# Moving a weight unit ahead of two others and a square ahead of a normalisation in a fused attention and mixing kernel

## The chip, the cores and the metric

The kernel runs on one core of a Trainium2 chip. Its engines are TensorE (matrix products, PE in the profile), VectorE (DVE), ScalarE (ACT), GpSimd (POOL) and SyncE (SP, which here only issues loads and stores). Each runs its own list of instructions in order, and they wait for each other through semaphores. The metric is the time of one execution on the device in microseconds; the median of three is given.

## The reference

Three parts follow one another. All of it is in float32.

```
scores = q @ k.T / sqrt(64); masked to a window of 32 keys (4 heads)
         or to every 4th of 128 keys (4 heads); attn = softmax; x = attn @ v
x_prev = x shifted by one token
xk = mu_k * x + (1 - mu_k) * x_prev ;  xr = mu_r * x + (1 - mu_r) * x_prev
k = relu(xk @ w_k) ; v = (k * k) @ w_v ; x = sigmoid(xr @ w_r) * v
u = x + (x.T @ U @ V).T ;  out = u + relu(u @ w_ch1) @ w_ch2
```

There are 4 batches of 576 tokens, 8 heads of 64, a width of 512, a hidden width of 1024 in the second part and 2048 in the third.

## The kernel before

A float32 product is made of three products of a format that TensorE takes faster: each operand is split into a high part and a low part (the rest), and high times high, high times low and low times high are added up. `three` (L1200) issues them. ScalarE makes most high parts, VectorE or GpSimd the low ones.

The attention is cut into 8 parts `k` of 256 or 320 tokens, and each part into 4 pairs of heads `p`. A pair goes through four steps: A transposes q and k (VectorE, L970 to L989); B makes the scores (TensorE), masks them and takes the negated maximum (VectorE, L999 to L1009); then ScalarE takes the exponentials (`exps`, L733) and VectorE divides by the sum (`normalise`, L1027); C transposes the probabilities (TensorE) and ScalarE copies them out of PSUM (L730); D multiplies by v (TensorE), and VectorE copies the result into x. Every step B, C and D takes a pair of PSUM banks. `GROUPS` (L117) is their order, and from part 1 on they use two bank pairs in turn (`TWO`, L121), so that a step waits until the step two places ahead of it has left its banks.

The second part runs over 9 chunks `c` of 256 tokens. A chunk has 10 units on TensorE (`UNITS`, L144): 8 k units (12 matmuls of 256 columns, for 128 hidden features each) and 2 r units (12 of 512 columns). ScalarE takes the relu of a k unit and its high square (`high_sq`, L806), in chunk 0 the plain square too, and VectorE the low part of the square (`square`, L1053). The product with w_v for the features m is called V m below (6 matmuls of 512 columns); `V_AFTER` (L145) says behind which unit it stands. A k unit waits until all units but the last are out of PSUM, and relu k m waits for the low square of k m-2.

A unit is also a slot: unit n of chunk c is slot 10 c + n, and `FIRST_ONE`, `SECOND_ONE` and `LATER` (L95 to L97) give the slots of the steps of part 1, part 2 and the later ones. On TensorE the steps of a slot stand behind its unit and its V (L1332), in the last slot ahead of V (L1317). Within a slot the order is A, C, B, D. ScalarE takes exps of a step B in the slot behind it, in two pieces around that slot's copies (L745 to L752). The r units take a sigmoid, for which ScalarE loads another function table, and it loads the table for exponentials again behind them.

The next chunk's input is made alongside: `shift` on ScalarE (L782), `mix` on VectorE (L1040), `mix_r` on GpSimd, in the slots `SHIFT_SLOT` and `MIX_SLOT`; `high_x` and `low_xk` (L1049, the low part of the whole k input) stand at the end of the chunk. Slots of chunk 0 wait for weights, which GpSimd splits in the order `PIECES1` (L164): k0 and k1, k2 and k3, both r halves, V0 and V1, k4 and k5, V2 and V3, and so on. GpSimd also makes the low parts of chunk 0's r input (L660), behind the first half of the w_v piece.

Ahead of chunk 0 comes the list `BEFORE` (L91): the steps of part 0 and B of part 1, pair 0. In between TensorE makes k0 and k1 by quarters as the inputs come (`first_unit`, L1367; a quarter is 3 matmuls). The third part (L1412) starts behind chunk 8 and isn't touched; it takes more than half of the time.

## Time and profile before

| | before |
|---|---|
| median of 3 runs | 775.22 us (775.13 to 776.5) |
| the profiled execution | 776.9 us |
| its span, first to last instruction | 774.9 us |
| PE busy | 749.9 us, 97% |
| DVE, ACT, POOL busy | 328.5, 297.3, 168.6 us |
| PE waits that the profile names, 20 to 76 us | 6.3 us |
| PE waits for sq_l (L1061), whole span | 3.2 us, 7 times |

A row of the timeline gives the start in microseconds from the start of the span, the duration, the engine, the line, the instruction with its operands and in brackets the idle time ahead of it with what ended it. The end of a matmul is modelled, so the cost of a group of matmuls is read from the start of one group to the start of the next.

### The profile page before, as it was taken

What the parts mean: (1) busy time and instruction counts of PE and PEld (TensorE: products, weight loads), DVE (VectorE), ACT (ScalarE), POOL (GpSimd) and SP (SyncE); (2) the same over time, 40 slices, a digit from 0 to 9 for tenths busy, and PEclk for the clock granted to TensorE, in tenths of its full rate; (3) what the DMA queues carried; (4) which work ended last, traced back from release to release, by engine and by line L of the source; (5) the groups of instructions that cost most, each with busy time, mean ns of one, the idle gap of its engine ahead of it and who ended that gap; (6) DMA issues with size and microseconds to landing.
All of it is one profiled execution on the core that took longest, in us unless ns stands there. A gap on an engine that the chain in (4) does not pass through costs nothing.

```text
span 774.9 us, 13327 instructions
## 1 busy us (share of the span) xinstructions
PE 749.9 (97%) x5020; PEld 654.8 (84%) x5020; DVE 328.5 (42%) x696; ACT 297.3 (38%) x785; POOL 168.6 (22%) x257
## 2 busy tenths in 40 slices
PE   4799999999999999999999999999999999999998
PEld 3588888888888887788899999998999999999987
DVE  6779675768576747746311311311131121113111
ACT  4777767676767655524331111111121111112110
POOL 6997020212021223404871000000000000000000
PEclk9999999999999999999999999999999999999999
DMA  7963432333232101001430100000010000001001
GB/s 146 207 171 70 84 72 40 60 62 63 45 66 54 42 1 55 1 28 56 136 135 1 41 1 0 29 13 0 0 41 0 0 15 25 0 0 41 0 1 41
DMA packets 121747, 35.76 MB, mean 46 GB/s; under 512 B 109536, under 2 KB 115680, under 8 KB 121696
## 3 DMA queue, kind: packets, MB, share of 16 engines
q1 hardware_dynamic: 112000, 34.02, 18.0%
q10 hardware_dynamic: 9696, 1.05, 0.9%
q8 instruction: 32, 0.52, 0.3%
q14 instruction: 19, 0.16, 0.1%
HBM read 30.33 MB, written 4.72 MB: 45 GB/s over the span
## 4 chain that ended last, share of the span: by engine, by line
PE 88%; DVE 7%; issue 2%; ACT 1%; DMA 1%; POOL 0%; ACTq 0%; DVEq 0%
PE bank L1202 27%; PE bank L1204 26%; PE bank L1203 26%; PE bank L1223 2%; PE bank L1254 2%; PE bank L1243 2%; PE bank L1283 1%; DVE probs L999 1%; PE bank L1349 1%; DVE sq_l L1061 1%; DVE neg_max L1009 1%; ACT probs L740 1%; DVE x L1021 1%; DVE sq L1057 1%; PE bank L1236 0%
## 5 line engine op out<-in xcount | busy, mean ns | idle before, releaser
L1172 DVE SCALAR_TENSOR_TENSOR h_l<-bank,h_h 128x384 fp32r<-128x384 f32 x96 | 53.5, 558 | 306.1 <-ACT h_h L938 306.1
L938 ACT ACTIVATE h_h<-bank 128x384 fp32r<-128x384 f32 x96 | 47.2, 491 | 326.3 <-PE bank L1204 326.3
L1202 PE MATMUL bank<-ut_h,w_h 128*128 128x384 f32 x384 | 130.5, 340 | 0.0
L1204 PE MATMUL bank<-ut_h,w_l 128*128 128x384 f32 x384 | 129.3, 337 | 0.0
L1203 PE MATMUL bank<-ut_l,w_h 128*128 128x384 f32 x384 | 128.8, 335 | 0.0
L1204 PE MATMUL bank<-w_h,h_l 128*128 128x512 f32 x288 | 113.7, 395 | 0.0
L1203 PE MATMUL bank<-w_l,h_h 128*128 128x512 f32 x288 | 113.5, 394 | 0.0
L1202 PE MATMUL bank<-w_h,h_h 128*128 128x512 f32 x288 | 112.0, 389 | 0.0
L1202 PE MATMUL bank<-xs_h,wk_h 128*128 128x256 f32 x288 | 86.9, 302 | 0.1
L1203 PE MATMUL bank<-xs_l,wk_h 128*128 128x256 f32 x288 | 81.8, 284 | 0.0
L1204 PE MATMUL bank<-xs_h,wk_l 128*128 128x256 f32 x288 | 81.7, 284 | 0.0
L1202 PEld LDWEIGHTS bank<-ut_h,w_h 128*128 128x128 f32 x384 | 72.2, 188 | 3.9 <-issue 0.8
L1203 PEld LDWEIGHTS bank<-ut_l,w_h 128*128 128x128 f32 x384 | 72.2, 188 | 3.0
L1204 PEld LDWEIGHTS bank<-ut_h,w_l 128*128 128x128 f32 x384 | 72.0, 188 | 0.0
L1204 PEld LDWEIGHTS bank<-w_h,h_l 128*128 128x128 f32 x288 | 54.0, 187 | 11.5
L1203 PEld LDWEIGHTS bank<-w_l,h_h 128*128 128x128 f32 x288 | 54.0, 188 | 9.5
L1202 PE MATMUL bank<-wv_h,sq_h 128*128 128x512 f32 x144 | 58.7, 407 | 3.4 <-DVE sq_l L1061 3.2
L1202 PEld LDWEIGHTS bank<-w_h,h_h 128*128 128x128 f32 x288 | 54.1, 188 | 9.0
L1202 PEld LDWEIGHTS bank<-xs_h,wk_h 128*128 128x128 f32 x288 | 55.6, 193 | 4.9 <-issue 2.3
L841 ACT ACTIVATE relu_k<-bank 128x256 f32<-128x256 f32 x72 | 26.9, 374 | 84.4 <-PE bank L1204 84.2
L1204 PE MATMUL bank<-wv_h,sq_l 128*128 128x512 f32 x144 | 56.9, 395 | 0.0
L1203 PE MATMUL bank<-wv_l,sq_h 128*128 128x512 f32 x144 | 56.9, 395 | 0.0
(119 smaller groups left out, 1224.9 us busy)
## 6 DMA issues: line engine op xcount, KB each, us to landing
stage<-in_moe_w_ch_dram SPq DMA_DIRECT2D x16, 512.0 KB, 3.3
out_dram<-result SPq DMA_DIRECT2D x18, 256.0 KB, 2.1
q_raw<-in_q_dram SPq DMA_DIRECT2D x64, 40.0 KB, 2.1
q_raw<-in_q_dram SPq DMA_DIRECT2D x64, 32.0 KB, 2.0
v_raw<-in_v_dram SPq DMA_DIRECT2D x32, 64.0 KB, 2.4
k_raw<-in_k_dram SPq DMA_DIRECT2D x48, 40.0 KB, 2.1
k_raw<-in_k_dram SPq DMA_DIRECT2D x52, 32.0 KB, 2.1
stage<-in_moe_w_k_dram SPq DMA_DIRECT2D x3, 512.0 KB, 4.4
```

Of the source, the lines that this page charges most:

```text
L740: ins = act.activation(probs[b][:, keys * i:keys * i + keys], probs[b][:, keys * i:keys * i + keys], ACT.Exp, bias=neg_max[:, b, i:i + 1], ...
L841: act.activation(relu_k[:, m % 2, :], unit_bank[n % 2][:, 0:C1], ACT.Relu).then_inc(unit_out, 1)
L938: act.activation(h_h[:, m % KRING, :], h_bank[m % 2][:, 0:C2], ACT.Relu).then_inc(hh_done, 1)
L999: ins = dve.scalar_tensor_tensor(probs[b][:, 0:4 * keys].rearrange("p (h c) -> p h c", h=2), banks[:, :, 0:2 * keys], DH ** -0.5, m[:, :, ...
L1009: dve.tensor_reduce(neg_max[:, b, 0:nu], probs[b][:, 0:nu * keys].rearrange("p (a b) -> p a b", b=keys), op=ALU.max, axis=AX_X, negate=Tru ...
L1172: dve.scalar_tensor_tensor(h_l[:, m % KRING, :], h_bank[m % 2][:, 0:C2], 0.0, h_h[:, m % KRING, :].bitcast(F32), op0=ALU.max, op1=ALU.subt ...
L1202: pe.matmul(dst, lhs[0], rhs[0], start=start, stop=False)
L1203: pe.matmul(dst, lhs[0], rhs[1], start=False, stop=False)
L1204: return pe.matmul(dst, lhs[1], rhs[0], start=False, stop=stop)
L1223: ins = pe.matmul(dst[UQ * a:UQ * a + UQ, h, col:col + keys], q_t[n % 2][rows, query:query + UQ], k_t[p][rows, first_key:first_key + keys] ...
L1243: ins = pe.transpose(run[0:keys, i * P:i * P + P], probs[n % 2][:, keys * i:keys * i + keys], ident[:, :])
L1254: ins = pe.matmul(run[rows, to:to + wide], v_raw[n % VALUES][0:keys, i + a, rows], probs_t[n % 2][0:keys, block_, first:first + wide], sta ...
```

## The change

In chunk 0 the unit k3 stands ahead of r0 and r1. V1 moves with r0 (slot 4), V2 goes behind k5. In slot 3 of chunk 0 the attention steps stand ahead of V0. The steps of part 1 move to later slots: B of pairs 1, 2 and 3 from slots 0, 1 and 3 to 2, 3 and 4; C from 1, 3, 4 and 5 to 2, 4, 5 and 6; D from 2, 4, 5 and 6 to 3, 5, 6 and 7; A of pair 3 from slot 1 to 2. The exponentials of part 1, pair 2 are taken at the end of slot 3, where B stands, so ahead of r0's sigmoid. Shifts and mixes of chunk 1's input move one slot later. Ahead of chunk 0, two quarters of k1 and one of k0 stand ahead of B(1,0); the high part and the low part of one quarter of the k input stand one step later; the exponentials of B(1,0) and the high parts of the r input move into chunk 0, behind unit 0 and behind unit 2; the loads of the keys of pairs 2 and 3 are issued sooner in ScalarE's list. In every chunk the square of k7 stands in slot 9 ahead of that slot's normalisation (in chunks 7 and 8 ahead of the token-mix steps), where it stood behind them.

```diff
-FIRST_ONE = {"A": [None, None, None, 1], "B": [None, 0, 1, 3], "C": [1, 3, 4, 5], "D": [2, 4, 5, 6]}
+FIRST_ONE = {"A": [None, None, None, 2], "B": [None, 2, 3, 4], "C": [2, 4, 5, 6], "D": [3, 5, 6, 7]}
+SOONER = (FIRST_ONE["B"][2], 1, 2)
...
-UNITS = [("k", 0), ("k", 1), ("k", 2), ("r", 0), ("r", 1), ("k", 3), ("k", 4), ("k", 5), ("k", 6), ("k", 7)]
-V_AFTER = [[], [], [], [0], [1], [2], [], [3], [4], [5, 6, 7]]
+UNITS = [("k", 0), ("k", 1), ("k", 2), ("k", 3), ("r", 0), ("r", 1), ("k", 4), ("k", 5), ("k", 6), ("k", 7)]
+V_AFTER = [[[], [], [], [0], [1], [], [], [2, 3], [4], [5, 6, 7]]] + [[[], [], [], [0], [1], [2], [], [3], [4], [5, 6, 7]]] * (NC1 - 1)
...
-SHIFT_SLOT = [[3, 5, 6, 7]] + [[1, 2, 5, 7]] * (NC1 - 2)
-MIX_SLOT = [[4, 6, 7, 8]] + [[2, 3, 6, 8]] * (NC1 - 2)
+SHIFT_SLOT = [[4, 6, 7, 8]] + [[1, 2, 5, 7]] * (NC1 - 2)
+MIX_SLOT = [[5, 7, 8, 9]] + [[2, 3, 6, 8]] * (NC1 - 2)
...
             def attention_slot(slot):
-                behind = [(k, p) for st, k, p in steps_in(slot - 1) if st == "B"] if slot else []
+                behind = [(k, p) for st, k, p in steps_in(slot - 1) if st == "B" and (k, p) != SOONER[1:]] if slot else []
...
+                if slot == SOONER[0]:
+                    exps(*SOONER[1:], 0)
+                    exps(*SOONER[1:], 1)
...
                         if c == 0 and n == 0:
+                            load_keys(1, 3)
+                            first_exps(1, 0)
+                        if c == 0 and n == 2:
                             high_first_r(0)
                             high_first_r(1)
...
-            high_first(1)
             attention("C", 0, 3)
             first_shift(2)
+            high_first(1)
             high_first(2)
             first_shift(3)
             high_first(3)
-            shift_for_r(0, 0)
-            shift_for_r(0, 1)
-            shift_for_r(0, 2)
-            load_keys(1, 2)
-            shift_for_r(0, 3)
-            first_exps(1, 0)
-            load_keys(1, 3)
+            for t in range(KT):
+                shift_for_r(0, t)
+                if t == 1:
+                    load_keys(1, 2)
...
+                        if n == NUNIT - 1:
+                            square(c, M1 - 1)
                         for k, p in normalised_in(slot + n):
                             if (k, p) != (1, 0):
                                 normalise(k, p)
                     else:
+                        if n == NUNIT - 1:
+                            square(c, M1 - 1)
                         for step in mix_steps("vector", (c - MIX_CHUNK) * NUNIT + n):
                             mix_step(*step)
-                square(c, M1 - 1)
...
+            mix(0, 2)
             low_first(1).then_inc(first_low, 1)
-            mix(0, 2)
...
-                    if n == NUNIT - 1:
+                    others_first = n == NUNIT - 1 or c == 0 and n == UNIT["k", KT - 1]
+                    if others_first:
                         other_work(c, n)
...
                     first_unit(1, 0)
                     first_unit(0, 1)
-            first_unit(1, 1)
-            first_unit(0, 2)
-            first_unit(1, 2)
+                    first_unit(1, 1)
+                    first_unit(0, 2)
+                    first_unit(1, 2)
```

## Rows read from the trace of the kernel before

**Rows 1.** The page: busy time by engine; the chain that ended last.

```profile
PE 749.9 (97%) x5020; PEld 654.8 (84%) x5020; DVE 328.5 (42%) x696; ACT 297.3 (38%) x785; POOL 168.6 (22%) x257
...
PE 88%; DVE 7%; issue 2%; ACT 1%; DMA 1%; POOL 0%; ACTq 0%; DVEq 0%
```

**Rows 2.** Busy time by stretch: stretch, length, engines with instructions, granted clock, DMA.

```profile
33.50:37.29 3.79, 2.33 (x32) 1.65 (x32) 3.03 (x9) 3.63 (x12) 3.71 (x6) 1.00 1.03 234
37.29:41.08 3.79, 3.79 (x33) 3.43 (x33) 2.93 (x7) 2.58 (x12) 3.71 (x7) 0.55 0.98 246
50.40:56.70 6.30, 5.93 (x54) 4.78 (x53) 3.94 (x8) 5.45 (x16) 6.14 (x9) 1.00 0.51 141
```

**Rows 3.** Timeline of TensorE in the lead-in and chunk 0.

```profile
28.89 0.92 PE L1223 MATMUL bank<-k_t,q_t 64*64 64x96 f32 x16 [1.71 <-DVE k_t L985]
...
35.55 0.72 PE L1243 MATMUL bank<-ident,probs 128*96 128x128 f32 x5 [0.44 <-DVE probs L1037]
...
38.39 0.58 PE L1202 MATMUL bank<-xs_h,wk_h 128*128 128x256 f32 x1
...
41.08 0.89 PE L1254 MATMUL bank<-probs_t,v_raw 96*64 96x64 f32 x24
...
50.40 0.40 PE L1202 MATMUL bank<-wv_h,sq_h 128*128 128x512 f32 x1
...
51.80 0.71 PE L1243 MATMUL bank<-ident,probs 128*96 128x128 f32 x5
...
54.77 0.40 PE L1202 MATMUL bank<-wv_h,sq_h 128*128 128x512 f32 x1
...
56.70 0.72 PE L1243 MATMUL bank<-ident,probs 128*96 128x128 f32 x5 [0.37 <-DVE probs L1037]
```

**Rows 4.** Timeline of ScalarE in chunk 0 (ACTq: loads that it issues).

```profile
33.63 0.51 ACTq L878 DMA_DIRECT2D k_raw<-in_k_dram  x1
...
34.18 0.38 ACT L841 ACTIVATE relu_k<-bank 128x256 f32<-128x256 f32 x1
...
35.23 1.14 ACT L804 ACTIVATE xs_h<-xf 128x512 fp32r<-128x512 f32 x2
...
51.21 1.28 ACT L740 ACT_TABLE_LOAD   x1
...
57.52 0.70 ACT L730 ACTIVATE probs_t<-bank 96x640 f32<-96x640 f32 x1 [1.41 <-PE bank L1243]
```

**Rows 5.** Timeline of VectorE in the lead-in and chunk 0.

```profile
24.77 0.99 DVE L1046 SCALAR_TENSOR_TENSOR xf<-x,mu,shifted 128x256 f32<-128x256 f32 x1 [0.56 <-ACT shifted L772]
...
36.25 0.56 DVE L999 SCALAR_TENSOR_TENSOR probs<-bank,mask_unit 128x384 f32<-128x384 f32 x1
...
39.15 0.51 DVE L977 STREAM_TRANSPOSE q_t<-q_raw 128x320 f32<-128x320 f32 x1 [0.82 <-DMA k_raw<-in_k_dram]
...
41.11 0.65 DVE L1009 TENSOR_REDUCE neg_max<-probs 128x5 f32<-128x480 f32 x1
```

**Rows 6.** Timeline of GpSimd in chunk 0.

```profile
37.33 2.97 POOL L660 TENSOR_TENSOR xs_l<-xf,xs_h 128x256 fp32r<-128x256 f32 x4
```

**Rows 7.** Waits of TensorE, 75 to 320 us: total, times, longest.

```profile
PE bank L1202 <- DVE sq_l L1061: 2.4, 5, 0.6
```

**Rows 8.** Timeline of VectorE at the ends of chunks 0 and 1.

```profile
73.21 1.75 DVE L1051 TENSOR_TENSOR xs_l<-xf,xs_h 128x1024 fp32r<-128x1024 f32 x1
...
108.83 0.19 DVE L1032 TENSOR_SCALAR sums<-sums 128x5 f32<-128x5 f32 x1
...
109.85 0.42 DVE L1057 TENSOR_TENSOR sq<-relu_k 128x256 f32<-128x256 f32 x1
...
110.65 1.22 DVE L1051 TENSOR_TENSOR xs_l<-xf,xs_h 128x1024 fp32r<-128x1024 f32 x1
```

**Rows 9.** Timeline of TensorE at the starts of chunks 1 and 2.

```profile
75.11 0.36 PE L1202 MATMUL bank<-xs_h,wk_h 128*128 128x256 f32 x1
...
112.28 0.28 PE L1202 MATMUL bank<-xs_h,wk_h 128*128 128x256 f32 x1
```

More of the change, by code:

```diff
@@ L1316, in chunk @@
                             turn(0, t)
-                    if n == NUNIT - 1:
+                    others_first = n == NUNIT - 1 or c == 0 and n == UNIT["k", KT - 1]
+                    if others_first:
                         other_work(c, n)
-                    for m2 in V_AFTER[n]:
+                    for m2 in V_AFTER[c][n]:
                         if m2 == 0:
@@ L1331, in chunk @@
                         ins.then_inc(v_mm, 1)
-                    if n < NUNIT - 1:
+                    if not others_first:
                         other_work(c, n)
```

## The prediction, made before the changed kernel was built

> **What bounds the kernel now.** I read the page first: TensorE is busy for 97% of the span and carries 88% of the chain that ended last [rows 1]. So only two things on TensorE move the end: time in which it stands idle, and time at its lower clock. Second, I read the busy time and the granted clock by stretch around chunk 0 [rows 2]. Idle there is 1.46 us in 33.50 to 37.29 and 0.37 us in 50.40 to 56.70. The clock is mostly at its lower level, 1.2 of 2.4 GHz, in 37.29 to 41.08, right after the stretch in which TensorE was busy for 2.33 of 3.79 us. Third, the timeline of TensorE gives the start of each step [rows 3], and those of ScalarE, VectorE and GpSimd what released it [rows 4 to 6]. Last, the waits of the chunks behind it: TensorE waits five times in 75 to 320 us for the low part of the last square, 2.4 us in all [rows 7], at the end of chunks 1 to 5.
>
> **Lead-in.** high_first(1) moves behind C(0,3)'s copy and one shift. In the old order VectorE ran low_first(1) inside a wait of 0.56 us ahead of mix(0,2) [rows 5]; now the low part (0.42 us) comes after mix(0,2), and everything behind it on VectorE comes about 0.4 us later: D(0,3), mix(0,3), A(1,0). B(1,0) then starts at about 29.3 us, not 28.89 [rows 3]. In return, nine of the first-unit matmuls now fill the 1.71 us wait ahead of B(1,0). That is a gain only if TensorE, and not the ScalarE and VectorE chain, is late next. It is the chain: shift_for_r, exps(1,0) and normalise(1,0) all stand 0.4 us later, so C(1,0) starts at 35.55 + 0.4 = 35.95. Unit k2 stands ahead of it and is done by about 33.5, so I expect some 2.4 us of idle there.
>
> **C(1,0) to D(1,0).** After C(1,0), B(1,1) takes TensorE to about 37.2. k3 follows and ends at 38.7 at the upper clock. At the lower clock a k unit takes 2.69 us (38.39 to 41.08, [rows 3]), and it ends near 39.9. With so little done between 33.5 and 37 I expect the lower clock, as in the old stretch of the same time. Then B(1,2), whose banks C(1,0)'s copy must have left. That copy now stands behind relu k2 with its squares, and relu k2 waits for VectorE's low square of k0. Normalise(1,0) and A(1,2) end near 36.6 and the low square near 37.0; relu k2 and its two squares take 1.05 us, as the same three of k0 did from 34.18 to 35.23 [rows 4]. So the copy runs 38.1 to 38.75. Then D(1,0), which needs the banks of B(1,1), that is VectorE's masking of it. VectorE did this at 36.25, ahead of A(1,3). Now A(1,3) stands ahead of it, and in the old trace A(1,3) waited until 39.15 for keys whose last issue was at 33.63 [rows 4, 5]. load_keys(1,3) now stands ahead of first_exps(1,0) and is freed by relu k0 at about 31.9, not 32.21, so keys land near 38.8. A(1,3) and a masking took 1.96 us (39.15 to 41.11, [rows 5]): the bank is free at 40.75. With k3 and B(1,2) at the lower clock TensorE gets there at about 40.9 as well, so two separate chains give D(1,0) at 40.95, not 41.08. The ends: 39.5 (keys early and upper clock) and 41.6.
> On the keys the Trainium skill has a rule: "Trainium Kernel Development and Optimization", section Key Constraints, says that DMAs from SP, ACT and POOL queues share the same 16 engines, and that another issuing engine saves only issue time. By that rule the keys would still land behind the same traffic; without it they would come with the 0.3 us by which they are issued sooner. The sum stands either way, because the matmuls alone give 40.9.
>
> **D(1,0) to C(1,3).** From D(1,0) to the end of r1 took 9.32 us (41.08 to 50.40, [rows 3]). V1 now stands inside it, 1.40 us (50.40 to 51.80, [rows 3]). r0 needs the low parts of the r half; GpSimd began them at 37.33 and takes 2.97 us [rows 6]. The high parts now come after C(1,0)'s copy at 38.75, so with half a microsecond for the first of them the low parts end near 42.25. r0 is wanted at 43.2: hidden by 0.9 us, and the bound if D(1,0) is early. GpSimd's splits come 1.9 us later; k4 then has its weights near 49, and wants them at 53. r1 ends at 40.95 + 9.32 + 1.40 = 51.67.
> The decisive step comes next. Behind r1's sigmoid ScalarE loads the exp table (1.28 us at 51.21, [rows 4]), runs exps(1,3), and VectorE normalises; the chain from the end of r1 to C(1,3) is 50.40 to 56.70 = 6.30 us [rows 3], and no instruction of it changes. Under it TensorE had V1 (1.40), C(1,2), D(1,1) and k3 (51.80 to 54.77, 2.97) and V2 (1.40), together 5.77. V1 has gone ahead, V2 has gone behind k5, k4 takes k3's place: 2.97 us of cover is left. TensorE must stand idle 3.3 us ahead of C(1,3), which starts at 51.67 + 6.30 = 57.97, against 56.70: +1.27. V2 and k4 have changed places, at 1.40 and 1.51, which leaves the rest of chunk 0 at the 18.41 us from 56.70 to chunk 1's first k0 at 75.11 [rows 3, 9].
> Behind it B(2,0) now stands between C(1,3) and D(1,2), so by the alternation of bank pairs D(1,2) needs C(1,3)'s copy. That copy started 0.82 us after C(1,3) and took 0.70 [rows 3, 4]; C(1,3) and B(2,0) last about 1.1: +0.5. Tail: shift and mix one slot later fall into waits; +0.1 at most. Without the clock chunk 0 ends 1.8 us later.
> **The clock.** A gap of 3.3 us followed by small matmuls is thinner than 33.50 to 37.29, where 1.46 us of idle was enough for the lower level behind it [rows 2]. A k unit at the lower level costs 2.69 - 1.51 = 1.2 us more. Part of the slow time can fall into the gap itself: between nothing and 1.4, and I take the middle, 0.7, as no row says how much falls into the gap. Chunk 0: +2.5 us.
> The Trainium skill's page "TensorE: Matmul & The Clock Gate", section Why this matters for your kernels, warns against idle gaps between bursts of matmuls because the clock then falls to half. By this rule the drop here is certain and the term is at its upper half, 0.7 to 1.4; if one holds that a single gap costs only its own length, it is nothing and chunk 0 ends at +1.8.
>
> **Chunks 1 to 8: square ahead of normalisation.** In chunk 1 the normalisation runs from 108.83 to 109.85, then the square and its low part until low_xk at 110.65 [rows 8]. Without these 1.02 us ahead of it the low square ends at 109.7, a quarter of a microsecond or more ahead of TensorE's need, since its longest wait there was under 0.8: the wait goes. But low_xk follows both, and ends at 110.65 + 1.22 = 111.87 as before [rows 8]. The next k0 needs it. At the end of chunk 0 k0 started 0.15 us after it (73.21 + 1.75 = 74.96, then 75.11, [rows 8, 9]); in chunk 1 k0 started at 112.28 [rows 9], 0.41 after. So k0 can come only 0.26 sooner, less 0.07 for its own restart. The five ends have 0.41 to 0.43 there: 5 x 0.2 = 1.0 us, with 0 and 1.4 as its ends. Chunk 6 has no normalisation there, and in chunk 7 the same order of VectorE's work leaves low_xk where it is: nothing. In chunk 8 the square delays one token-mix addition and the low parts of u by 0.7 us, hidden behind V5 to V7.
>
> **Sum.** +2.5 - 1.0 = +1.5 us. The profiled execution took 776.9 with a span of 774.9, so its successor should show 778.4 and 776.4; the median of the runs was 775.22, 1.7 lower than the profiled one. I forecast 776.7 us.
>
> **Rivals.** (1) The chain between r1 and C(1,3) is shortened or D(1,0) comes at 39.5: r0 is then held by the low parts to 42.4, r1 ends at 50.9, 0.8 sooner, and with no drop of the clock chunk 0 ends at +1.0; the boundaries give 1.4: 774.8. Only if VectorE's work also shortens would it be under 773.7. For it: the keys took over 5 us to land (33.63 to 39.15, [rows 4, 5]), so other traffic sets it, and an issue 0.3 us sooner may gain more than that. Against: the fixed 6.30 us.
> (2) Slower still: the lower clock meets V0 and r0 as well. It decides if k2 to B(1,2) are so thin that the clock comes back only after D(1,0); then another 1.4 to 2 us of dense work is slow, and the boundaries still give 1.0: 778.4. For it: 2.4 us of idle at 33.5, more than the old trace had there. Against: k3 and B(1,2) are back to back.
> (3) The early filling does what it says: the nine matmuls (2.0 us at the lower clock's 0.22 each, 12 of them being 2.69) and an earlier rise of the clock reach the path in full, because exps(1,0) is not late. Then all of chunk 0 comes out 1 us sooner, and with the boundaries the kernel takes 773.2.
>
> **How the numbers follow.** Forecast (775.6 to 777.6): 0.48. Rival 1: 0.20. Rival 2: 0.19. Rival 3: 0.13. The range reaches from rival 3's upper part to rival 2: 773.6 to 778.5. A difference under 0.2%, 1.55 us, can't be told from no change here. Slower by more (over 776.77): half of the forecast and rival 2, 0.43. Faster by more (under 773.67): most of rival 3 and a little of rival 1, 0.14. Within: 0.43.
>
> **What would show it.** Idle of about 3.3 us of TensorE ahead of C(1,3), released by VectorE's L1037, and one of 2 us or more ahead of C(1,0); V1 between r0 and C(1,1) with no wait; B(1,1)'s masking behind A(1,3); the granted clock below 1 behind C(1,3); no TensorE wait for sq_l at the ends of chunks 1 to 5, and a new, shorter one for low_xk (L1051). Wrong would be: C(1,3) at 56.7 or sooner, or chunk 1's first k0 before 75.1.

## The result, and the profile after

The changed kernel took 781.14 us (median of 5 runs, 780.91 to 782.96) against 775.22 us for the kernel before: a ratio of 1.0078, 95% interval 1.0063 to 1.0092. It is 5.9 us slower; the forecast was 776.7 us and the range ended at 778.5. Its profiled execution took 781.14 us, so it is the median one, with a span of 779.1 us.

Engines by busy time (page of the kernel after, to be read beside [rows 1]): TensorE worked 1.5 us longer, though it has the same 5020 matmuls, and its share of the chain went down by one point, to 87%.

```profile
PE 751.4 (96%) x5020; PEld 656.2 (84%) x5020; DVE 325.8 (42%) x696; ACT 296.8 (38%) x785; POOL 167.2 (21%) x257
...
PE 87%; DVE 7%; ACT 2%; issue 1%; DMA 1%; POOL 0%; ACTq 0%; DVEq 0%
```

Busy time by stretch of the kernel after (stretch, its length, busy time with instructions of TensorE, its weight loads, VectorE, ScalarE and GpSimd, granted clock, DMA share, GB/s). The first two stretches answer to the first two of [rows 2]. The third runs from the end of r1 to C(1,3), as the last of [rows 2] does, and the next two from there to chunk 1's first k0.

```profile
33.94:37.30 3.36, 0.00 (x0) 0.03 (x1) 1.17 (x4) 2.89 (x13) 1.74 (x4) 1.00 1.07 249
37.30:42.51 5.21, 5.21 (x61) 4.42 (x62) 5.13 (x11) 3.53 (x9) 3.30 (x6) 0.67 0.91 264
...
53.23:59.45 6.22, 3.30 (x42) 2.77 (x42) 4.82 (x10) 5.36 (x16) 5.98 (x9) 0.99 0.63 159
59.45:66.00 6.55, 6.33 (x55) 5.55 (x55) 3.74 (x7) 2.08 (x5) 6.31 (x10) 0.50 0.35 62
66.00:79.92 13.92, 13.92 (x132) 11.67 (x131) 7.82 (x20) 10.57 (x34) 5.92 (x10) 1.00 0.37 67
```

Two holes, and behind each a stretch at a lower clock. TensorE does nothing at all from 33.94 to 37.30 and works 3.30 of 6.22 us ahead of C(1,3), where it worked 5.93 of 6.30. Behind the second hole the clock is 0.50, all of it the lower level, for 6.6 us; the kernel before had 1.00 there.

The timeline of TensorE after gives the steps that answer to [rows 3], and the first k0 of chunks 1 and 2, as in [rows 9].

```profile
37.30 0.72 PE L1251 MATMUL bank<-ident,probs 128*96 128x128 f32 x5 [3.38 <-DVE probs L1042]
...
42.51 0.89 PE L1262 MATMUL bank<-probs_t,v_raw 96*64 96x64 f32 x24
...
54.06 0.72 PE L1251 MATMUL bank<-ident,probs 128*96 128x128 f32 x5 [0.67 <-DVE probs L1042]
...
59.45 1.27 PE L1251 MATMUL bank<-ident,probs 128*96 128x128 f32 x5 [2.26 <-DVE probs L1042]
...
79.92 0.28 PE L1210 MATMUL bank<-xs_h,wk_h 128*128 128x256 f32 x1
...
116.44 0.35 PE L1210 MATMUL bank<-xs_h,wk_h 128*128 128x256 f32 x1 [0.40 <-DVE xs_l L1056]
```

C(1,0), C(1,2) and C(1,3) all wait for probabilities that VectorE has normalised. Chunk 1 starts at 79.92 instead of 75.11: +4.81 us. From there to the end it takes 779.1 - 79.92 = 699.18 instead of 774.9 - 75.11 = 699.79 us: -0.6. Together +4.2, the difference of the two profiled spans. The other 1.7 us of the 5.9 lie between the profiled execution of before (776.9) and its median (775.22); E6 below shows where most of them probably come from.

Waits of TensorE after, 82 to 345 us (total, times, longest), against [rows 7] and the 3.2 us in seven waits for sq_l of the table ahead of the prediction:

```profile
PE bank L1210 <- DVE xs_l L1056: 2.0, 6, 0.4
PE bank L1210 <- DVE sq_l L1066: 0.7, 1, 0.7
```

The waits for the low square are gone at six ends, and six for low_xk stand in their place. Of the 0.6 us that the chunks behind chunk 0 give back, chunks 1 to 5 give 0.8; chunk 6 is 0.3 us longer than before (33.43 instead of 33.16 us), also in E5, and no run shows why.

### The profile page after: what moved, and what is told of

Same layout as the page of the kernel before. It is cut to its first block, busy times and chain, and to the rows that moved or that the text cites. A ratio compares the mean times of both kernels' runs of the same rounds, so it can differ in the third digit from the quotient of the medians.

```text
span 779.1 us, 13327 instructions
## 1 busy us (share of the span) xinstructions
PE 751.4 (96%) x5020; PEld 656.2 (84%) x5020; DVE 325.8 (42%) x696; ACT 296.8 (38%) x785; POOL 167.2 (21%) x257
## 2 busy tenths in 40 slices
DMA packets 121747, 35.76 MB, mean 46 GB/s; under 512 B 109536, under 2 KB 115680, under 8 KB 121696
## 4 chain that ended last, share of the span: by engine, by line
PE 87%; DVE 7%; ACT 2%; issue 1%; DMA 1%; POOL 0%; ACTq 0%; DVEq 0%
PE bank L1210 27%; PE bank L1212 26%; PE bank L1211 26%; PE bank L1251 2%; PE bank L1262 2%; PE bank L1231 2%; PE bank L1291 1%; DVE xs_l L1056 1%; PE bank L1358 1%; ACT probs L742 1%; DVE probs L1042 1%; DVE probs L1004 1%; DVE sq_l L1066 1%; DVE sq L1062 1%; POOL w_l L623 0%
## 5 line engine op out<-in xcount | busy, mean ns | idle before, releaser
L1211 PEld LDWEIGHTS bank<-xs_l,wk_h 128*128 128x128 f32 x288 | 56.2, 195 | 0.9
```

Source lines behind the costliest of these rows:

```text
L1211: pe.matmul(dst, lhs[0], rhs[1], start=False, stop=False)
```

## The experiments

The theory after this reading (T): +5.9 is made of the cover taken from under the chain r1, exps(1,3), C(1,3), with the clock falling behind the hole; of a late C(1,0); and of a fall of the clock behind C(1,0). The square ahead gives back 0.6 to 1. Rivals: the hole costs only its own length; the moved steps make their own delays wherever V1 and V2 stand; the first hole alone decides the clock of the front.

All ratios are against the kernel before on the same chips (median 775.1 to 775.3). Where a kernel and the changed one have overlapping intervals, their difference is not settled by the times, and the trace is used.

| kernel | median us (range) | ratio, 95% interval | C(1,0) | D(1,0) | C(1,3) | chunk 1's k0 |
|---|---|---|---|---|---|---|
| before | 775.1 to 775.3 | 1 | 35.55 | 41.08 | 56.70 | 75.11 |
| after | 781.14 (780.91 to 782.96) | 1.0078, 1.0063 to 1.0092 | 37.30 | 42.51 | 59.45 | 79.92 |
| E1 keys behind | 780.11 (778.58 to 781.11) | 1.0071, 1.0054 to 1.0087 | 35.76 | 40.93 | 58.18 | 77.61 |
| E2 cover back | 776.85 (775.48 to 777.79) | 1.0019, 1.0010 to 1.0029 | 38.19 | 44.41 | 60.08 | 76.59 |
| E3 both back | 775.04 (773.98 to 776.35) | 0.9995, 0.9981 to 1.0008 | 36.24 | 41.38 | 57.09 | 73.61 |
| E4 more work in the second hole | 780.19 (779.26 to 781.03) | 1.0063, 1.0046 to 1.0080 | 37.88 | 44.40 | 61.70 | 79.80 |
| E5 without the square part | 781.60 (780.75 to 782.68) | 1.0090, 1.0073 to 1.0107 | 37.38 | 42.52 | 59.56 | 78.97 |
| E6 before + square ahead | 775.01 (773.25 to 776.84) | 0.9997, 0.9984 to 1.0011 | 35.53 | 39.51 | 55.39 | 73.00 |
| E7 before + square, low_xk ahead | 771.26 (770.43 to 772.55) | 0.9950, 0.9932 to 0.9967 | 35.33 | 39.32 | 55.63 | 73.22 |
| E8 before + lead-in part | 776.73 (775.07 to 777.80) | 1.0006, 0.9991 to 1.0021 | 36.50 | 40.42 | 56.67 | 75.08 |
| E9 more work in the first hole | 779.49 (777.14 to 780.78) | 1.0054, 1.0039 to 1.0069 | 37.18 | 41.44 | 58.14 | 76.05 |
| E10 more work in both | 779.42 (778.59 to 779.90) | 1.0046, 1.0030 to 1.0062 | 38.55 | 42.29 | 60.14 | 78.47 |
| E11 E3 + low_xk ahead | 771.92 (770.91 to 774.33) | 0.9956, 0.9942 to 0.9971 | 36.70 | 40.87 | 56.46 | 72.98 |
| E12 V2 alone back | 778.37 (776.92 to 779.45) | 1.0033, 1.0019 to 1.0047 | 38.00 | 44.20 | 61.29 | 77.80 |

The last four columns are starts in each kernel's profiled execution, in us. Executions of one kernel differ (those of before on these chips took 774.05 to 779.73 us), and in chunk 0 in part by whether the clock fell there, so a single start says less than a median. The mean clock quoted below is that of a whole execution, of which each result gives one number.

**E1: the keys' loads issued behind the exponentials again.** In chunk 0, slot 0:

```diff
-                            load_keys(1, 3)
                             first_exps(1, 0)
+                            load_keys(1, 3)
```

> The changed kernel with one pair of calls swapped: load_keys(1, 3) stands behind first_exps(1, 0) in ScalarE's list, not ahead of it. Theory: in the changed kernel the four load issues (32.23 to 34.08 us) hold ScalarE's instruction list, so exps(1,0) begins at 34.13, 1.5 us after the square of k0; here it begins at about 32.6, C(1,0) at 35.9 instead of 37.30, and C(1,3) 0.9 to 1.4 us sooner: 779.7 to 780.2 us. Rival: D(1,0) is held by the masking behind A(1,3), whose keys now are issued later than in the changed kernel, so D(1,0) stays at 42.5 or comes later and the kernel takes 781.1 us or more.

ScalarE after, around the place (ACTq: loads that it issues):

```profile
32.23 0.32 ACTq L886 DMA_DIRECT2D k_raw<-in_k_dram  x1
32.55 0.40 ACT L816 ACTIVATE sq<-relu_k 128x256 f32<-128x256 f32 x1
32.58 1.50 ACTq L886 DMA_DIRECT2D k_raw<-in_k_dram  x3
34.13 0.37 ACT L742 ACTIVATE probs<-probs,neg_max 128x96 f32<-128x96 f32 x1 [1.18 <-issue]
```

and in E1:

```profile
31.89 0.40 ACT L816 ACTIVATE sq<-relu_k 128x256 f32<-128x256 f32 x1
32.06 0.32 ACTq L886 DMA_DIRECT2D k_raw<-in_k_dram  x1
32.19 0.36 ACT L742 ACTIVATE probs<-probs,neg_max 128x96 f32<-128x96 f32 x1
32.41 0.51 ACTq L886 DMA_DIRECT2D k_raw<-in_k_dram  x1
```

After the change, the four issues take ScalarE's list from 32.23 to 34.08, and the first exponential, whose scores have long been there, starts at 34.13: "1.18 <-issue". In E1 the issues run beside the exponentials, which are already with the engine. C(1,0) comes 1.54 us sooner, and the kernel takes 780.11 us, as the theory had it. The two medians alone do not separate E1 from the changed kernel; E3 against E2, the same edit with the cover in place, does: 775.04 against 776.85 with intervals that don't meet, 1.8 us.

The clock falls behind the second hole here too, though TensorE's hole is longer (2.94 us) than in the changed kernel's profile (2.26), but for about half as long. Stretches of E1 behind C(1,3), against 59.45:66.00 after:

```profile
58.18:60.75 2.57, 2.11 (x42) 1.68 (x43) 1.77 (x5) 1.75 (x4) 2.41 (x5) 0.92 0.58 100
60.75:64.00 3.25, 3.25 (x15) 3.11 (x16) 1.76 (x3) 0.59 (x3) 3.17 (x5) 0.54 0.42 82
```

**E2: V1 and V2 back under the chain.** V1 stands behind r1 and V2 behind k4, as they stood behind r1 and k3 before:

```diff
-V_AFTER = [[[], [], [], [0], [1], [], [], [2, 3], [4], [5, 6, 7]]] + ...
+V_AFTER = [[[], [], [], [0], [], [1], [2], [3], [4], [5, 6, 7]]] + ...
```

> The changed kernel with V1 behind r1 (not r0) and V2 behind k4 (not k5), so that both stand under the chain from r1's end over the table load and exps(1,3) to C(1,3). Theory: the idle time ahead of C(1,2) and C(1,3), 0.67 and 2.26 us, goes nearly in full, 2.8 us of work comes out of the path, and with the gap the lower clock behind C(1,3) goes too (about 2.5 us): 776.0 us. If the gap counts but the clock doesn't follow it: 778.3 us. Rival: ScalarE and VectorE are the bound all through chunk 0 and the idle time only moves to other places: 780 us or more.

The kernel takes 776.85 us, 4.3 us less than the changed one, for 776.0 foreseen. TensorE's hole ahead of C(1,3) shrinks to 0.42 us, and no lower clock follows; the front hole is as large as ever (3.61 us) and has its lower clock behind it, twice as long as in the changed kernel's profile (timeline and stretches of E2):

```profile
38.19 1.06 PE L1251 MATMUL bank<-ident,probs 128*96 128x128 f32 x4 [3.61 <-DVE probs L1042]
...
60.08 0.72 PE L1251 MATMUL bank<-ident,probs 128*96 128x128 f32 x5 [0.42 <-DVE probs L1042]
```

```profile
38.00:42.00 4.00, 3.81 (x35) 2.96 (x36) 2.62 (x8) 2.71 (x6) 1.05 (x2) 0.50 1.06 278
42.00:46.00 4.00, 4.00 (x55) 3.52 (x55) 3.24 (x9) 2.31 (x11) 3.92 (x7) 0.75 0.45 81
60.08:66.00 5.92, 5.46 (x83) 4.46 (x84) 3.47 (x7) 3.78 (x12) 5.68 (x9) 1.00 0.33 59
```

So the cover is the largest part of the loss, and the rival that the moved steps delay themselves wherever V1 and V2 stand is out. The mean clock is 0.995 to 0.998 in all ten executions, though nothing falls behind C(1,3) in the profile: in the changed kernel's order the fall in front is the rule.

**E3: E1 and E2 together.** Both diffs above.

> The changed kernel with both edits at once: the key loads behind first_exps(1, 0), and V1 behind r1 and V2 behind k4. Each alone gave 780.11 and 776.85 us, against 781.14 of the changed kernel. Theory (two separate delays on one path): their gains add, 1.0 and 4.3 us: 775.8 us. Rival: once C(1,3) is covered the front of the chunk no longer matters (or the clock falls there anyway): 776.9 us.

775.04 us, for 775.8 foreseen, and level with the kernel before. What else the change does (k3 ahead of the r units, later slots, the lead-in, the square) is, taken together, worth nothing that can be measured; single parts may still cancel. The two edits together give back 6.1 us, a little more than 1.0 + 4.3.

**E4: the second hole filled with work.** k4 of chunk 0 is made three times, 24 more matmuls ahead of C(1,3); the sums are the same, as each starts afresh:

```diff
+                            for again in range(3 if c == 0 and m == 4 else 1):
                                 for t in range(KT):
                                     ins = three(dst[:, 0:C1], ...
```

> The changed kernel with TensorE making unit k4 of chunk 0 three times instead of once (24 matmuls more, about 2.8 us of them, same result), just where it stands idle ahead of C(1,3). Theory of the clock: the gap makes the granted clock fall behind C(1,3), where the matmuls of 59.4 to 66.2 us cost about 2.9 us more than at the upper level; with the gap filled the clock stays up and the kernel takes 778.3 to 779.0 us although it does more work. Rival: the fall has another cause (small matmuls of the attention steps alone): the clock falls all the same and the kernel takes 781 to 782 us.

With 24 more matmuls the kernel was not slower: 780.19, 0.95 us below the changed kernel with overlapping intervals, and between what the theory (778.3 to 779.0) and the rival (781 to 782) foresaw. Stretches of E4, from C(1,3) on, against 59.45 to 79.92 after:

```profile
61.70:68.58 6.88, 6.24 (x65) 5.04 (x65) 3.32 (x7) 5.51 (x19) 6.64 (x11) 1.00 0.29 53
68.58:79.80 11.22, 11.22 (x122) 9.73 (x122) 8.07 (x20) 8.10 (x23) 4.36 (x8) 1.00 0.38 68
```

From C(1,3) to k0 took 18.10 us in place of 20.47, with the same instructions: 2.4 us is the price of the lower clock behind the hole in the changed kernel's profile. Part of it is spent again on the added work, which is longer than the hole: 2.8 us at 0.116 each, in 2.26. And this execution, the slowest of its four, had a worse front: its granted clock was 0.50 from 38 to 44 us, and D(1,0) came 1.9 us later than after the change.

**E5: the changed kernel without its square part.**

```diff
-                        if n == NUNIT - 1:
-                            square(c, M1 - 1)
...
+                square(c, M1 - 1)
```

> The changed kernel without its last part: the square of k7 stands again behind the normalisation and the token-mix steps. Theory (the square ahead gains 0.2 us at each of five chunk ends, since low_xk is next): TensorE's waits for sq_l come back at chunks 1 to 5, those for low_xk go, 782.1 us. Rival: low_xk takes all back, 781.1 us. Second rival: the wait is worth its full length, 0.5 to 0.7 us each: 784 us.

781.6 against 781.14: 0.5 us in the direction foreseen, but the intervals overlap.

**E6: the square part alone, on the kernel before.** The same edit the other way round.

> The kernel before with one part of the change alone: the square of k7 ahead of the normalisation (and of the token-mix steps in the last two chunks). Theory: the wait for sq_l (0.3 to 0.6 us, five chunk ends) goes and a wait for low_xk of 0.2 to 0.4 us takes its place, net 0.2 us each: 774.2 us. Rival: the full length of the waits with their restarts, 0.5 to 0.7 us each: 772.1 us. Second rival: nothing left after low_xk: 775.2 us.

775.01 us, a ratio of 0.9997: nothing to be measured. The trace shows a small gain. Chunk 0's last slot, from V5 to the next k0, took 4.88 us before and takes 4.30, as its two waits are gone. Of the chunks behind it, those that end with a normalisation of five tiles become 0.2 to 0.3 us shorter, those with one of four tiles 0.04: 0.8 us in chunks 1 to 5. At the short ends the low square, now earlier, runs beside GpSimd's low parts (VectorE, then GpSimd, of E6):

```profile
142.54 0.55 DVE L1057 TENSOR_TENSOR sq<-relu_k 128x256 f32<-128x256 f32 x1
143.12 0.84 DVE L1061 TENSOR_TENSOR sq_l<-sq,sq_h 128x256 fp32r<-128x256 f32 x1
```

```profile
140.68 3.01 POOL L643 TENSOR_TENSOR xs_l<-xf,xs_h 128x256 fp32r<-128x256 f32 x4 [2.23 <-ACT xs_h L791]
```

and in the kernel before, when GpSimd was done at 145.81 (VectorE, then GpSimd):

```profile
146.46 0.43 DVE L1061 TENSOR_TENSOR sq_l<-sq,sq_h 128x256 fp32r<-128x256 f32 x1
```

```profile
142.99 2.82 POOL L643 TENSOR_TENSOR xs_l<-xf,xs_h 128x256 fp32r<-128x256 f32 x4 [2.24 <-ACT xs_h L791]
```

0.84 against 0.43 us for the same subtraction. The Trainium skill, "SBUF — State Buffer", section "SBUF: two separate sides", says that a VectorE operation with two inputs in SBUF and a GpSimd operation that reads SBUF exclude each other for a whole instruction. The rows fit it: the excess of 0.41 us is less than one of GpSimd's four instructions (3.01 / 4 = 0.75).

E6 also tells where the profiled execution of before stood. Up to the last slot of chunk 0 its code is that of before. Stretches of E6 that answer to the first two of [rows 2]:

```profile
33.50:37.27 3.77, 2.09 (x32) 1.40 (x33) 3.05 (x9) 3.65 (x12) 2.88 (x6) 1.00 1.14 261
37.27:41.00 3.73, 3.31 (x57) 2.98 (x58) 3.65 (x8) 3.06 (x14) 3.73 (x6) 1.00 0.97 285
```

The first stretch is as thin as before's, and the second has its full clock, where before's profiled execution had 0.55. D(1,0) starts at 39.51 instead of 41.08. E7's profile shows the same (39.32). At C(1,3) 1.3 and 1.1 us of that are left (55.39 and 55.63 instead of 56.70).

**E7: low_xk ahead of the normalisation too.** On the kernel before, in chunks 0 to 6:

```diff
+                        if n == NUNIT - 1:
+                            square(c, M1 - 1)
+                            low_xk(c + 1)
                         for k, p in normalised_in(slot + n):
...
-                square(c, M1 - 1)
+                if c >= MIX_CHUNK:
+                    square(c, M1 - 1)
                 if last:
                     low_u(0)
-                else:
+                elif c == MIX_CHUNK:
                     low_xk(c + 1)
```

> The kernel before, with the square of k7 and low_xk of chunks 0 to 6 both ahead of the last slot's normalisation (nothing else moved; chunks 7 and 8 as before). Theory (low_xk is what is late once the square stands ahead): low_xk then ends near 110.9 in chunk 1, before V7 ends at 111.5, so neither wait is left, and the normalisation, some 1.2 us later, is still ahead of C(k,1) behind the next k0. Five ends give 0.5 to 0.7 us each, chunk 0's end 0.4: 771.8 us. Rival: the normalisation is late for C(k,1) and the waits only change their place: 774.2 us or more.

771.26 us, 0.9950 of the kernel before, 4.0 us faster. VectorE of E7 at the end of chunk 1, against [rows 8]:

```profile
107.32 0.42 DVE L1061 TENSOR_TENSOR sq_l<-sq,sq_h 128x256 fp32r<-128x256 f32 x1
107.66 1.22 DVE L1051 TENSOR_TENSOR xs_l<-xf,xs_h 128x1024 fp32r<-128x1024 f32 x1
108.80 0.16 DVE L1032 TENSOR_SCALAR sums<-sums 128x5 f32<-128x5 f32 x1
```

low_xk ends at 108.88 instead of 111.87; its chunk 1 began 1.9 us sooner, so 1.1 us of that is the edit. TensorE's waits of E7 from 77 to 345 us come down to one line:

```profile
PE bank L1206 <- DVE sq_l L1061: 0.8, 2, 0.7
```

The same five chunks in which the square alone gave 0.8 us in the trace give 3.7 here. This is the fastest kernel of the study.

**E8: the lead-in part alone, on the kernel before.** The two quarters of k1 and one of k0 ahead of B(1,0), high_first(1) and low_first(1) one step later.

> The kernel before with the lead-in part of the change alone: first_unit(1,1), (0,2) and (1,2) ahead of B(1,0), high_first(1) behind C(0,3)'s copy and the next shift, low_first(1) behind mix(0,2). Theory: the path of this stretch is the chain over VectorE and ScalarE, which comes 0.1 to 0.4 us later, and the nine matmuls ahead of B(1,0) gain nothing or only what stands between B(1,0) and B(1,1): 774.5 to 775.6 us. Rival: filling the wait pays in full, 2 us, and with a sooner rise of the clock more: 773.2 us or less.

776.73 us. The ratio, 1.0006 with an interval of 0.9991 to 1.0021, doesn't separate it from the kernel before; its median is 1.6 us above that of the kernel before on this chip (775.14), so a cost of 1 us or more isn't excluded, and the gain of the rival is. C(1,0) started at 36.50 in its profile, 0.95 later than before, for 0.4 foreseen. TensorE now stands idle for 2.64 us ahead of B(1,1), and the clock falls behind that:

```profile
34.41:38.17 3.76, 3.36 (x32) 2.40 (x32) 2.98 (x9) 3.58 (x12) 3.68 (x6) 0.55 0.97 230
```

The mean clock is 0.993 to 0.998 in all twelve executions; in 19 of 29 of the kernel before on the same chip it is 0.999 or 1.000. So the lead-in part alone makes the fall in front more frequent. In E3, which contains it, five of ten executions have 0.999 or more.

**E9: the first hole filled.** As E4, with `m == 2`: 24 more matmuls ahead of C(1,0).

> The changed kernel with TensorE making unit k2 of chunk 0 three times (24 matmuls more, about 2.8 us, same result), where it stands idle ahead of C(1,0) (33.9 to 37.3 us in the changed kernel). Theory: that idle lets the granted clock fall for C(1,0), B(1,1) and k3 (38.7 to 42.3 us at the lower level); filled, k3 takes 1.5 us and not 2.8, D(1,0) waits only for the masking behind A(1,3) at about 41.5 and comes 1 us sooner: 780.1 us. Rival: D(1,0) is held by ScalarE and VectorE alone: 781.1 us or, if the added matmuls delay C(1,0), more.

779.49 us, for 780.1 foreseen: 1.65 below the changed kernel with more to do, the intervals overlapping a little. In the profile the clock stays up over the whole of chunk 0, also behind the second hole, which is still there (timeline and stretches of E9):

```profile
58.14 0.72 PE L1251 MATMUL bank<-ident,probs 128*96 128x128 f32 x5 [2.01 <-DVE probs L1042]
```

```profile
37.18:41.44 4.26, 3.77 (x62) 3.01 (x62) 3.22 (x10) 3.13 (x8) 2.91 (x5) 1.00 0.76 198
...
58.14:66.00 7.86, 7.40 (x102) 6.06 (x102) 4.00 (x9) 5.53 (x18) 7.62 (x12) 1.00 0.54 119
```

So a hole of 2 us ahead of C(1,3) does not always bring the clock down: in this execution it didn't, in the profiled one of the changed kernel it did. E9's profiled execution, 777.14 us, is its fastest of ten; the slowest took 780.78. Three executions have a mean clock of 0.999 or 1.000 and took 777.14 to 777.87 us; the other seven have 0.993 to 0.998 and took 779.28 to 780.78. Which executions fall is open. As both holes kept the clock here, with only the first one filled, the rival that the first hole decides for both is neither shown nor out.

**E10: both holes filled.**

> The changed kernel with both k2 and k4 of chunk 0 made three times (48 matmuls more). Filling the gap ahead of C(1,3) alone gave 780.19 us. Theory (the clock is lost in both gaps, and each loss is separate): the granted clock is 1.0 from 34 us on, and the time is the sum of both gains, about 1 us each: 779.1 us. Rival: the waits for ScalarE and VectorE set the end of chunk 0 and the clock is only a part that they hide: 780.2 us or more.

779.42 us, between the theory and the rival, and not less than E9, so the two fillings don't add. The profile shows why. The clock is kept, as in E9's profile: its mean was 0.999 to 1.000 in all nine executions, so what is left of the loss is not the clock. And in this execution the four key loads held ScalarE's list much longer (ScalarE of E10):

```profile
32.31 3.03 ACTq L886 DMA_DIRECT2D k_raw<-in_k_dram  x3
35.38 0.38 ACT L742 ACTIVATE probs<-probs,neg_max 128x96 f32<-128x96 f32 x1 [2.71 <-issue]
```

three issues in 3.03 us, where the changed kernel's took 1.50, and C(1,0) is 1.25 us later. The price of issues ahead of an urgent instruction is not fixed. Ahead of C(1,3) the added 2.8 us also overfill the hole.

**E11: E3 with low_xk ahead as well.**

> The changed kernel with the key loads behind first_exps(1, 0), V1 behind r1, V2 behind k4 (775.04 us with these), and low_xk of chunks 0 to 6 ahead of the last slot's normalisation as well. Theory: low_xk ahead gives here what it gives on the kernel before, in the chunks 1 to 5 0.6 us each and at chunk 0's end 0.2 to 0.4, less the 0.7 us that the square alone has brought already: 775.0 - 3.1 = 771.9 us, level with the kernel before with the same order (771.26). Rival: the lead-in and the new order of the units are worth something once the waits are gone: 770.5 us or less.

771.92 against 771.26 for E7, with overlapping intervals: the repaired change and the kernel before are worth the same with this edit on top.

**E12: V2 alone back behind k4.**

```diff
-V_AFTER = [[[], [], [], [0], [1], [], [], [2, 3], [4], [5, 6, 7]]] + ...
+V_AFTER = [[[], [], [], [0], [1], [], [2], [3], [4], [5, 6, 7]]] + ...
```

> The changed kernel with V2 alone put back behind k4 (V1 stays behind r0), so half of the cover ahead of C(1,3) is back: of 2.9 us of idle 1.5 us stay. If only idle time counts: 781.1 - 1.4 = 779.7 us. If the clock falls behind C(1,3) only with the long gap: another 2.4 us, 777.4 us. If the gap left is still enough for the fall: 779.7 us with the granted clock at 0.5 behind C(1,3).

778.37 us: 2.8 of the 4.3 us of E2 come back with one of the two products. Timeline and stretches of E12:

```profile
61.29 0.72 PE L1251 MATMUL bank<-ident,probs 128*96 128x128 f32 x5 [1.44 <-DVE probs L1042]
```

```profile
55.08:61.29 6.21, 4.55 (x47) 3.77 (x48) 4.36 (x10) 5.36 (x16) 5.97 (x9) 1.00 0.56 136
61.29:66.00 4.71, 4.25 (x57) 3.72 (x58) 3.49 (x7) 2.57 (x6) 4.55 (x7) 1.00 0.29 54
```

Between r1 and C(1,3) TensorE is idle for 1.66 us in place of 2.92, and the clock stays up behind it. V2's cover is worth its own 1.3 us and about as much again, which the clock would explain but which no run separates; V1's is worth the remaining 1.5 us.

## Why the prediction was wrong

The steps, as starts in us. "Clean" is E9, which has the changed kernel's order and no lower clock in chunk 0, beside E6, which has the order of before and none either.

| step | forecast | after | E6 | E9 | E9 - E6 |
|---|---|---|---|---|---|
| C(1,0) | 35.95 | 37.30 | 35.53 | 37.18 | +1.65 |
| D(1,0) | 40.95 | 42.51 | 39.51 | 41.44 | +1.93 |
| C(1,3) | 57.97 | 59.45 | 55.39 | 58.14 | +2.75 |
| chunk 1's k0 | 77.61 | 79.92 | 73.00 | 76.05 | +3.05 |

(77.61 is 75.11 + 2.5.) The changed kernel's chunk 0 ends 6.92 us later than E6's: 3.05 by waiting, and 79.92 - 76.05 = 3.87 by the clock, of which 1.3 ahead of C(1,3) and 20.47 - 17.91 = 2.56 behind it. The split rests on three single executions.

Against the forecast the miss is 781.14 - 776.7 = 4.4 us: 79.92 - 77.61 = 2.3 in chunk 0, 1.7 in the baseline, 0.4 in the boundaries.

**Lead-in: the place right, the reason for C(1,0) short by 1.35 us.** B(1,0) at 29.3 was 29.15, and the nine matmuls gained nothing, as E8 shows. The failed step is "load_keys(1,3) now stands ahead of first_exps(1,0) ... so keys land near 38.8". It counts what the loads gain by going sooner and not what they hold up: four issues in ScalarE's list, 1.85 us (E1). The row to see it by was there: an issue of 0.51 us in [rows 4]. As to the gain, the last issue stood at 33.6 us as before, so it wasn't sooner at all. It landed 3.5 us later instead of 5.4, at about 37.1, but by other traffic and for nothing: A(1,3) ran at 39.50 without a wait, since VectorE's list reached it only then. So the keys bounded nothing here, and the issue time was what counted. The rule of the Trainium skill that stood beside this step ("Trainium Kernel Development and Optimization", Key Constraints), that another issuing engine saves only issue time, fits the trace: with issues at the same moment the landing differed by 1.9 us. What the prediction left out is that the issue time is also spent somewhere.

**C(1,0) to D(1,0): right apart from its start.** Forecast 5.00 us, measured 5.21, at a clock of 0.67. Of the two chains only the one over the matmuls bounded it: the masking ended at 41.4, and in E9, at full clock, D(1,0) waits for it until 41.44.

**D(1,0) to the end of r1: right.** Forecast 9.32 + 1.40 = 10.72, measured 42.51 to 53.22 = 10.71, and V1 with no wait.

**r1 to C(1,3): right.** Forecast 6.30, measured 6.22; forecast idle 3.3, measured 2.26 ahead of C(1,3) and 0.67 ahead of C(1,2), together 2.9. E2 shows that it decides.

**The clock: the mechanism right, the term mis-sized.** The step is "between nothing and 1.4, and I take the middle, 0.7". In the changed kernel's profile it was 2.4 (against E4) to 2.56 (against E9) behind C(1,3). The only price behind the bound of 1.4 is 1.2 us for one k unit at the lower level, but C(1,3), B(2,0), D(1,2), a k unit and the start of V2 all ran at it: 6.55 us at 0.50. A ceiling taken from one unit holds only if the slow stretch is one unit long, and no row said so. The rule of the Trainium skill's page "TensorE: Matmul & The Clock Gate" (Why this matters for your kernels), weighed there, would have put the term at its upper half, 0.7 to 1.4: the direction was right, and in this profile it was still more than 1 us short. That the drop is certain isn't borne out: E9 has none behind a hole of 2.01 us. Nor was the 1.46 us of [rows 2] enough by itself: E6 was idle for 1.68 us in the same stretch and kept the clock. The size isn't fixed either: in the profiles of E1 and E5 C(1,3) to k0 took 19.43 and 19.41 us, so the same term is 1.5 there, behind holes of 2.94 and 2.81 us. Against this stands a stretch that was 1.1 us too dear: the forecast without the clock is 18.41 + 0.6 = 19.0, and E9 took 17.91. The wait of D(1,2) for C(1,3)'s copy was sized rightly (0.46 us in E9, 0.21 after, where the matmuls ahead of it are slow). But the 18.41 contains chunk 0's last slot with its two waits for VectorE, 4.88 us, and those aren't there after the change (4.29, also in E5 without the square part): 0.6 us. The other 0.5 isn't traced to one step. So in the sum only 0.8 us shows.

**The baseline: a step that wasn't in the sum at all.** The prediction took 1.7 us off the forecast, as the profiled execution of before was 1.7 above its median. But what lifted it is, for the most part, the fall of the clock at 37.29 to 41.08 [rows 2]. E6 and E7, with the same code there, have none, and their C(1,3) is 1.1 to 1.3 us sooner (D(1,0) 1.6 to 1.8). The rest is open: executions of before with a mean clock of 1.000 took 774.05 to 777.29 us. The prediction carried that stretch into the changed kernel as given, "as in the old stretch of the same time", and then subtracted the 1.7 as well. It can't be both. In most executions of before (54 of 76 in the later measurements) the mean clock is 0.999 to 1.000, but in none of the twelve of E8, which adds only the lead-in, and in none of the ten of E2: in the changed kernel's order the slow front is the rule, before it the exception. The changed kernel's own 0.991 to 0.996 contain the second fall as well. Without taking the fall's 1.1 to 1.3 us off, the same sum gives 777.8 to 778.0; without taking off any of the 1.7, 778.4.

**Boundaries: right in place, 0.6 in size.** Forecast -1.0 (0 to -1.4), trace -0.6, times -0.5 (E5) and -0.2 (E6), which can't be told from nothing. The new waits for low_xk came as foreseen at chunks 1 to 5, and a sixth of 0.15 us at the end of chunk 7, together 2.0 us; the short ends, where GpSimd is in the way of the low square (E6), had been counted like the long ones; in the changed kernel the chunks that end with them are even 0.1 us longer than before, also without the square part (E5). That low_xk was the next in line is confirmed by E7.

**Rivals.** Rival 1 and rival 3 (774.8 and 773.2) are out: C(1,3) wasn't earlier, and the early filling gave nothing. Half of rival 3's mechanism did happen. Before, the matmuls of k0 and k1 stand 0.21 us apart until 33 us, which is their pace at the lower clock; after, B(1,0) at 29.15 already takes 0.49 us instead of 0.85 to the start of its second group, and the matmuls of k1 behind it stand 0.12 us apart. The time went into the waits for relu k0 (1.34 us) and ahead of C(1,0) (3.38 us), as exps(1,0) was no sooner. Rival 2 (778.4) named a right cause, more of the lower clock, at the wrong hole: V0 at 43.33 ran at full clock again, and the long slow stretch stood behind C(1,3). Slower was given 0.43, as much as no change. The range ended too early because it took one mishap at a time: the issues, the longer slow stretch and the baseline came together.

## What to carry to other kernels

A load issued from ScalarE's list costs it the issue time, here 0.3 to 0.5 us each and in one execution 1 us. Put it behind the urgent instruction, where it runs beside it, and not ahead.

Before filler work is moved, write down the longest fixed chain and what covers it: here V1, V2 and k3 under the 6.3 us from r1 to C(1,3). A hole on TensorE is to be priced at its own length plus what may run at the lower clock behind it, here 1.5 to 2.6 us or nothing. Work moved ahead into a wait gains nothing if the chain behind is late, and the wait that it leaves behind it can bring the clock down (E8). And where a profiled execution lies above its median, find the stretch that does it before either number is used.

An instruction moved ahead pays only as far as the next one in line: the square alone 0.2% at best, the square and low_xk together 0.5%.

## What the runs showed of the hardware

More work was not more time. 24 extra matmuls in a hole left the kernel at 780.19 (E4) and 779.49 (E9), with 781.14 without them.

A hole brings the clock down in some profiles and not in others. Ahead of C(1,3), 2.26 us of idle had a clock of 0.50 behind it for 6.6 us after the change; 2.94 us in E1 and 2.81 us in E5 had a lower stretch about half as long; 2.01 us in E9 and 1.44 us in E12 had 1.00. The length of the hole doesn't order them. They differ also in what stood 20 us earlier: E9 had no fall in front, and E12, like E2 and E4, had one that lasted twice as long as the changed kernel's. Each is one profile, and what decides stays open. That E4, E12 and E2 kept the clock because their hole was filled or shorter is therefore likely and not shown.

The column of the granted clock doesn't show all of TensorE's pace. From 28.00 to 33.50 us of the kernel before it reads 1.00, while the matmuls of 256 columns stand 0.21 us apart as they do at 0.50:

```profile
28.00:33.50 5.50, 4.25 (x37) 3.52 (x37) 3.84 (x11) 4.53 (x15) 5.34 (x9) 1.00 0.78 182
```

```profile
30.81 0.41 PE L1204 MATMUL bank<-xs_h,wk_l 128*128 128x256 f32 x1
31.02 0.41 PE L1202 MATMUL bank<-xs_h,wk_h 128*128 128x256 f32 x1
```

Three loads issued from ScalarE took 1.50 us in most profiles and 3.03 in one (E10), which has the same issues in the same place.
